# Whole rows by one indirect transfer, turned by sixteen VectorE transposes of 32 partitions

## The chip, the cores and the metric

The kernel runs on one core of one Trainium2 chip. The metric is device time in microseconds (us), the median of several runs. Engines are named as in the profile: PE is TensorE (its matmuls), PEld its weight loads, DVE is VectorE, ACT is ScalarE, POOL is GpSimd, SP is SyncE.

## The reference, cut to what matters

Three stages follow one another: a decaying linear attention, a dense feed-forward layer, and a layer of eight experts of which each token takes one. The change touches the third.

```python
x = attention(q, k, v, lam)                      # 1536 tokens x 512
h = x @ moe_w_in                                 # 512 -> 2048
x2 = np.maximum(0.01 * h, h) @ moe_w_out         # 2048 -> 512

logits = x2 @ w_gate + modality_bias[modality_id]
e_idx = np.argmax(logits, axis=1)                # one of 8 experts for each token
gate_w = softmax(logits)[np.arange(N), e_idx]
for e in range(8):
    mask = e_idx == e
    h = np.maximum(x2[mask] @ w1[e], 0.0)        # 512 -> 1024
    out[mask] = gate_w[mask, None] * (h @ w2[e]) # 1024 -> 512
```

Everything is 32-bit. Each large product is made of three matmuls, since every operand is split into a high part and the rest: `lo x hi`, `hi x lo` and `hi x hi`.

## The kernel before, in words

**Dense stage.** The 1536 tokens are three blocks of 512. For each block, 16 slices of 128 hidden features run through `layer1` and `layer2` on PE (12 matmuls of 128x512 each). Per slice, ACT makes the high parts of the weights (`split_in`, `split_out`) and of the activations (`hidden`), POOL the low parts of the weights, DVE the leaky ReLU and the low part of the activations (`leaky`). In the second half of the last block ACT and DVE also split the first expert's weights (`we_hi`, `we_lo`, L854 and L1219), one of 8 pieces per slice. The rows of x2 of a finished block are stored to DRAM, in `x2_d` (the profile calls it x_d); the router (`route`, `gates`, `slots`, `scatter_slots`) writes token numbers into `slots_d`, sorted by expert. `take` and `order` sort the experts.

**Expert stage.** It works on tiles of 128 tokens of one expert; here there are twelve, numbered 0 to 11, and three leftovers of at most 32 tokens of different experts, which are done together at the end (the mixed rows, names ending in `_m`). The first three tiles (`PRE`) belong to the first expert and take only tokens of the first two blocks; they are prepared while the dense stage ends. A tile t goes through this chain:

1. ACT's queue loads the token numbers (`load_rows`, L879), from tile 3 on.
2. POOL turns them into row addresses and issues the indirect transfer of the rows into `xg` (`gather`, `gather_early`).
3. DVE turns the rows so that features lie on the partitions, from `xg` into PSUM bank 6 (`turn_rows`, semaphore `s_et`).
4. ACT copies the high part out (`rows`, L800), DVE makes the low part (`rows_lo`, L1121).
5. PE multiplies: `up` twice (halves of 512 hidden features, 12 matmuls each), `turn_hidden` twice (L1493), `down` twice (12 matmuls each). ACT and DVE take the hidden features between them (`relu`, `hid`), DVE scales the result (`evacuate`) and POOL scatters it.

There is one `xg`, one bank for the turned rows, one `ids_n`. So tile t+1 can be gathered only after tile t is turned, and turned only after the low part of tile t is made. Each engine's order is written out by hand. On PE one body of the loop is `down(t, 0)`, `turn_hidden(t, 1)`, `up(t+1, 0)`, `down(t, 1)`, `turn_hidden(t+1, 0)`, `up(t+1, 1)`. On DVE it is `rows_lo(t+1)`, `hid(t, 1)`, `evacuate(t)`, `hid(t+1, 0)`, `turn_rows(t+2)`; in the body in which a new whole expert begins, sixteen halves of its weights' low parts are shared between DVE and POOL besides.

**Why the transpose is one instruction.** DVE's transpose turns blocks of 32x32 inside each group of 32 partitions. A full turn of 128 rows also has to bring rows of one partition group into another. The kernel before has the transfer do it: `x2_d` has four rows of 128 features for each token, one for each partition group, and the address of the row that partition p takes is four times the token number plus p // 32 (the constant `quarter`):

```python
pool.indirect_dma_start(out=xg[:, g * P:(g + 1) * P], ..., ap=ids_g[:, g:g + 1] ...)   # for g in 0..3
nc.vector.transpose(bank(T_PS).rearrange("p (c g j) -> p g c j", c=DC, g=QS),
                    xg[:].rearrange("p (g c i) -> p g c i", g=QS, c=DC))
```

For each g the 32 tokens of group g stand in all four partition groups, each time with another 128 of their features. That takes four indirect transfers of 128 pieces of 512 bytes, and four loads of token numbers.

Of the kernel before, what the change touches and what calls it, by code (L numbers as in the profile page):

```python
# [5 lines left out]
ALU = mybir.AluOpType  # L6
# [48 lines left out]
def fused_program(nc, attn_qk, attn_kv, lam, w_dense, modality, w_gate, mod_bias, w_exp, out):  # L55
# [6 lines left out]
    with ctx:  # L62
# [8 lines left out]
        x2_d = nc.dram_tensor("x2_d", [(TOK + 1) * QS, P], F32).ap()  # L71
        x2_rows = x2_d.rearrange("(t a) c -> t (a c)", a=QS)
# [103 lines left out]
        xg_m = place("xg_m", [P, MIX, P], F32)  # L176
# [15 lines left out]
        quarter = sb("quarter", [P, 1], F32)  # L192
# [29 lines left out]
        at_m = sb("at_m", [P, MIX], I32)  # L222
        at_m4 = sb("at_m4", [P, MIX], I32)
# [20 lines left out]
        at_pre = sb("at_pre", [P, PRE * QS], I32)  # L244
        at_pre4 = sb("at_pre4", [P, PRE * QS], I32)
        ids_n = sb("ids_n", [P, QS], I32)
        ids_g = sb("ids_g", [P, QS], I32)
# [4 lines left out]
        def bank(i):  # L252
            return psum[:, i, :]
# [143 lines left out]
        def _(sp):  # L397
# [84 lines left out]
            for t in range(BLOCKS):  # L482
# [3 lines left out]
                if t == BLOCKS - 1:  # L486
# [7 lines left out]
                    with nc.allow_non_contiguous_dma(reason="one id each"):  # L494
                        for a in range(QS):
                            sp.dma_start(at_pre[a * QR:(a + 1) * QR, :],
                                         slots_d[bass.ds(e_first * TOK, PRE * P), 0:1].rearrange("(g j) b -> j (g b)", j=QR)
                                         ).then_inc(s_idp, 16)
                sp.wait_ge(s_xr, DC * (t + 1))
                for a in range(QS):  # L500
                    sp.dma_start(x2_d[t * BLK * QS:(t + 1) * BLK * QS, :].rearrange("(b j a) n -> a j b n", a=QS, j=QR)[a],
                                 x2_r[a * QR:(a + 1) * QR].rearrange("p b c i -> p b (c i)")).then_inc(s_x2st, 16)
# [12 lines left out]
            for q in range(MIX):  # L515
                at = sp.value_load(m_tab[0:1, PLACES + q:PLACES + q + 1], min_val=0, max_val=SLOTS)
                sp.dma_start(ids_m[q * MR:(q + 1) * MR, :], slots_d[bass.ds(at, MR), :]).then_inc(s_mids, 16)
                with nc.allow_non_contiguous_dma(reason="one id each"):
# [23 lines left out]
        def _(pool):  # L542
# [14 lines left out]
            pool.dma_start(x2_rows[TOK:TOK + 1, :], zrow[:]).then_inc(s_out, 16)  # L557
# [56 lines left out]
            def gather_early(t):  # L614
                for g in range(QS):
                    pool.indirect_dma_start(out=xg[:, g * P:(g + 1) * P], out_offset=None, in_=x2_d[0:SURE * QS, :],
# [1075 lines left out]
```

## Time and profile before

| | |
|---|---|
| median of 3 runs | 521.85 us (521.41 to 525.5) |
| the profiled execution's own time | 522.88 us |
| its span in the trace | 521.0 us |
| PE busy | 484.8 us, 93% of the span |
| DVE busy | 202.9 us, 39% |
| ACT busy | 180.0 us, 35% |
| POOL busy | 247.8 us, 48% |
| mean granted TensorE clock | 0.982 of full speed |
| expert stage | from 329 us to the end |

The span runs from the first to the last instruction, and all times inside the program count from its start; the execution's own time holds 1.9 us more. A group in the profile is a line of the kernel with its engine and operation; where a row of the trace says `[x <-y]`, the engine sat idle for x us before it and y released it. The granted clock is 1.00 at 2.4 GHz and 0.50 at 1.2 GHz.

### The profile page before, as it was taken

What the parts mean: (1) busy time and instruction counts of PE and PEld (TensorE: products, weight loads), DVE (VectorE), ACT (ScalarE), POOL (GpSimd) and SP (SyncE); (2) the same over time, 40 slices, a digit from 0 to 9 for tenths busy, and PEclk for the clock granted to TensorE, in tenths of its full rate; (3) what the DMA queues carried; (4) which work ended last, traced back from release to release, by engine and by line L of the source; (5) the groups of instructions that cost most, each with busy time, mean ns of one, the idle gap of its engine ahead of it and who ended that gap; (6) DMA issues with size and microseconds to landing.
All of it is one profiled execution on the core that took longest, in us unless ns stands there. A gap on an engine that the chain in (4) does not pass through costs nothing.

```text
span 521.0 us, 8733 instructions
## 1 busy us (share of the span) xinstructions
PE 484.8 (93%) x2826; PEld 388.1 (74%) x2827; DVE 202.9 (39%) x434; ACT 180.0 (35%) x308; POOL 247.8 (48%) x265
## 2 busy tenths in 40 slices
PE   7899999999999999999999998879997988999991
PEld 6778888888778888877888886667775766888740
DVE  3533232333365422224632566466222372222210
ACT  0233334234354344445345555222221361222100
POOL 3874664554334556444446747361645175444300
PEclk9999999999999999999999999989998999999996
DMA  6954534321030620004700000400277728411100
GB/s 200 407 224 161 163 126 158 132 107 16 0 82 0 215 109 0 0 0 109 295 0 1 1 0 20 102 21 22 61 255 240 261 48 299 104 41 41 41 19 3
DMA packets 35433, 53.16 MB, mean 102 GB/s; under 512 B 15703, under 2 KB 23519, under 8 KB 35408
## 3 DMA queue, kind: packets, MB, share of 16 engines
q1 hardware_dynamic: 24576, 46.04, 26.7%
q0 software_dynamic: 3200, 6.77, 4.0%
q10 hardware_dynamic: 7632, 0.04, 0.8%
q8 instruction: 14, 0.23, 0.2%
q14 instruction: 11, 0.09, 0.1%
HBM read 46.41 MB, written 6.61 MB: 102 GB/s over the span
## 4 chain that ended last, share of the span: by engine, by line
PE 69%; DMA 7%; issue 7%; DVE 6%; ACT 4%; POOL 3%; ACTq 2%; POOLq 0%; SPq 0%; DVEq 0%
PE psum L1419 8%; PE psum L1427 7%; PE psum L1421 7%; PE psum L1420 7%; PE psum L1429 7%; PE psum L1428 7%; PE psum L1503 2%; PE psum L1382 2%; PE psum L1505 2%; PE psum L1504 2%; PE psum L1483 2%; PE psum L1377 2%; PE psum L1360 2%; PE psum L1485 2%; PE psum L1484 2%
## 5 line engine op out<-in xcount | busy, mean ns | idle before, releaser
L595 POOL TENSOR_TENSOR wi_lo<-wd_raw,wi_hi 128x512 fp32r<-128x512 f32 x48 | 62.1, 1294 | 138.2 <-ACT wi_hi L759 138.1
L1427 PE MATMUL psum<-act_lo,wo_hi 128*128 128x512 f32 x192 | 75.6, 394 | 2.4 <-DVE act_lo L1021 2.4
L1419 PE MATMUL psum<-xT,wi_lo 128*128 128x512 f32 x192 | 76.6, 399 | 0.0
L1421 PE MATMUL psum<-xT,wi_hi 128*128 128x512 f32 x192 | 74.9, 390 | 0.0
L1420 PE MATMUL psum<-xT,wi_hi 128*128 128x512 f32 x192 | 74.8, 390 | 0.0
L1429 PE MATMUL psum<-act_hi,wo_hi 128*128 128x512 f32 x192 | 74.8, 389 | 0.0
L1428 PE MATMUL psum<-act_hi,wo_lo 128*128 128x512 f32 x192 | 74.7, 389 | 0.0
L1018 DVE SCALAR_TENSOR_TENSOR act_f<-psum,act_f 128x512 f32<-128x512 f32 x48 | 33.1, 690 | 96.5 <-ACT act_f L777 96.0
L600 POOL TENSOR_TENSOR wo_lo<-wd_raw,wo_hi 128x512 fp32r<-128x512 f32 x48 | 61.9, 1289 | 1.0 <-ACT wo_hi L764 1.0
L777 ACT ACTIVATE act_f<-psum 128x512 f32<-128x512 f32 x48 | 28.7, 597 | 97.3 <-PE psum L1421 93.4
L696 POOL DMA_INDIRECT xg<-x_d,ids_g x40 | 41.0, 1025 | 18.4 <-issue 8.8
L1021 DVE TENSOR_TENSOR act_lo<-act_f,act_hi 128x512 fp32r<-128x512 f32 x48 | 35.5, 739 | 33.6 <-ACT act_hi L779 33.6
L1483 PE MATMUL psum<-we_hi,xe_lo 128*128 128x512 f32 x96 | 41.0, 427 | 6.1 <-DVE xe_lo L1121 4.2
L1427 PEld LDWEIGHTS psum<-act_lo,wo_hi 128*128 128x128 f32 x192 | 36.0, 188 | 12.6 <-issue 3.0
L779 ACT ACTIVATE act_hi<-act_f 128x512 fp32r<-128x512 f32 x48 | 30.4, 634 | 42.9 <-DVE act_f L1018 42.9
L1419 PEld LDWEIGHTS psum<-xT,wi_lo 128*128 128x128 f32 x192 | 36.0, 188 | 8.3
L1503 PE MATMUL psum<-we_hi,he_lo 128*128 128x512 f32 x96 | 38.8, 404 | 3.5 <-POOL we_lo L709 2.3
L1421 PEld LDWEIGHTS psum<-xT,wi_hi 128*128 128x128 f32 x192 | 36.0, 188 | 7.7
L1429 PEld LDWEIGHTS psum<-act_hi,wo_hi 128*128 128x128 f32 x192 | 36.0, 188 | 7.6
L1428 PEld LDWEIGHTS psum<-act_hi,wo_lo 128*128 128x128 f32 x192 | 36.1, 188 | 7.3
L1420 PEld LDWEIGHTS psum<-xT,wi_hi 128*128 128x128 f32 x192 | 36.1, 188 | 7.0
L1485 PE MATMUL psum<-we_hi,xe_hi 128*128 128x512 f32 x96 | 38.7, 403 | 0.0
(207 smaller groups left out, 742.4 us busy)
## 6 DMA issues: line engine op xcount, KB each, us to landing
we_raw<-w_exp SPq DMA_DIRECT2D x40, 512.0 KB, 5.2
wd_raw<-w_dense SPq DMA_DIRECT2D x16, 512.0 KB, 6.2
qk_in<-attn_qk SPq DMA_DIRECT2D x10, 512.0 KB, 3.4
kv_in<-attn_kv SPq DMA_DIRECT2D x10, 512.0 KB, 3.4
x_d<-x_r SPq DMA_DIRECT2D x12, 256.0 KB
qk_more<-attn_qk SPq DMA_DIRECT2D x2, 512.0 KB, 7.0
kv_more<-attn_kv SPq DMA_DIRECT2D x2, 512.0 KB, 7.8
ids_n<-slots_d ACTq DMA_DIRECT2D x44, 0.5 KB
```

The costliest lines, as they stand in the source:

```text
L595: nc.gpsimd.tensor_tensor(wi_lo[:, r, :], dense_raw(f, 0), wi_hi[:, r, :].bitcast(F32), ALU.subtract).then_inc(s_wil, 1)
L600: nc.gpsimd.tensor_tensor(wo_lo[:, r, :], dense_raw(f, 1), wo_hi[:, r, :].bitcast(F32), ALU.subtract).then_inc(s_wol, 1)
L696: pool.indirect_dma_start(out=xg[:, g * P:(g + 1) * P], out_offset=None, in_=x2_d, in_offset=bass.IndirectOffsetOnAxis(ap=ids_g[:, g:g + 1 ...
L1419: nc.tensor.matmul(h, w_lo, hi, start=(c == 0), stop=False)
L1420: nc.tensor.matmul(h, w_hi, lo, start=False, stop=False)
L1421: mm = nc.tensor.matmul(h, w_hi, hi, start=False, stop=(c == DC - 1))
L1427: nc.tensor.matmul(bank(ACC + c), hi, act_lo[:, r, :], start=first, stop=False)
L1428: nc.tensor.matmul(bank(ACC + c), lo, act_hi[:, r, :], start=False, stop=False)
L1429: return nc.tensor.matmul(bank(ACC + c), hi, act_hi[:, r, :], start=False, stop=last)
L1483: nc.tensor.matmul(bank(HID + half), xe_lo[:, c, :], w_hi, start=(c == 0), stop=False)
L1485: mm = nc.tensor.matmul(bank(HID + half), xe_hi[:, c, :], w_hi, start=False, stop=(c == DC - 1))
L1503: nc.tensor.matmul(bank(ACC), he_lo[:, f, :], we_hi[:, f, DM:], start=(f == 0), stop=False)
```

## The change

- `x2_d` has one row of 512 features for each token again. One indirect transfer of 128 pieces of 2 KB takes the place of four (also in `gather_early` and for the mixed rows), one load of token numbers takes the place of four, and a copy takes the place of the address arithmetic.
- `turn_rows` is sixteen transposes (`square`), each from one group of 32 partitions, g, to another, a. For the mixed rows it is twelve.
- The turn of tile 0 is moved into the last slices of the dense stage in two halves, `rows(0)` and `rows_lo(0)` before the last piece of the first expert's weights. Tile 1's turn is in two halves too, around `route` and `hid(0, 0)`.
- POOL issues the gather of tile 0 after the low parts that belong to slice 11; it stood ahead of the last low part of `wo` before.
- SP loads the weights of later experts once the gather of tile 3 is in; it no longer waits for token numbers too.

```diff
@@ SP
-                    with nc.allow_non_contiguous_dma(reason="one id each"):
-                        for a in range(QS):
-                            sp.dma_start(at_pre[a * QR:(a + 1) * QR, :], ...).then_inc(s_idp, 16)
...
-                    for a in range(QS):
-                        sp.dma_start(at_m[a * QR:(a + 1) * QR, q:q + 1], slots_d[bass.ds(at, MR), 0:1]).then_inc(s_mids, 16)
-
-            sp.wait_ge(s_gat, LOADS * (PRE + 1))
-            sp.wait_ge(s_ids, LOADS * (PRE + 1))
+            sp.wait_ge(s_gat, 16 * (PRE + 1))
@@ POOL
             def gather_early(t):
-                for g in range(QS):
-                    pool.indirect_dma_start(out=xg[:, g * P:(g + 1) * P], out_offset=None, in_=x2_d[0:SURE * QS, :], ...
+                pool.indirect_dma_start(out=xg[:], out_offset=None, in_=x2_d[0:SURE, :],
+                                        in_offset=bass.IndirectOffsetOnAxis(ap=ids_pre[:, t, 0:1].bitcast(U32), axis=0),
...
-            pool.wait_ge(s_x2st, LOADS * (BLOCKS - 1))
-            pool.wait_ge(s_chain, 8)
-            pool.wait_ge(s_idp, 16 + LOADS)
-            nc.gpsimd.tensor_scalar(at_pre4[:], at_pre[:], float(QS), quarter[:], ALU.mult, ALU.add).then_inc(s_chain, 1)
-            pool.wait_ge(s_chain, 9)
-            gather_early(0)
+            for i in range(FC1 - 6, FC1 - 2):
+                n = FC1 * (BLOCKS - 1) + i
+                split_in(n + 2, i + 2, i % 2)
+                split_out(n + 1, i + 1, 1 - i % 2)
+                if i == FC1 - 5:
+                    pool.wait_ge(s_x2st, LOADS * (BLOCKS - 1))
+                    pool.wait_ge(s_chain, 8)
+                    pool.wait_ge(s_idp, 16)
+                    gather_early(0)
             split_out(FC1 * BLOCKS - 1, FC1 - 1, 1)
...
             def gather(t):
-                nc.gpsimd.tensor_scalar(ids_g[:], ids_n[:], float(QS), quarter[:], ALU.mult, ALU.add).then_inc(s_idc, 1)
+                nc.gpsimd.tensor_copy(ids_g[:], ids_n[:]).then_inc(s_idc, 1)
...
-                for g in range(QS):
-                    pool.indirect_dma_start(out=xg[:, g * P:(g + 1) * P], out_offset=None, in_=x2_d, ...
+                pool.indirect_dma_start(out=xg[:], out_offset=None, in_=x2_d, ...
@@ ACT, last block, slices 8 to 15
                         hidden(n, i % 2)
+                        if i == FC1 - 1:
+                            rows(0)
                         ...
                         nc.scalar.activation(we_hi[:, f, :], we_raw[:, 0, f, :], ACT.Copy).then_inc(s_fh, 1)
-                    rows(0)
@@ DVE
-            def turn_rows(t):
-                dve.wait_ge(s_gat, LOADS * t + LOADS)
-                dve.sem_inc(s_pass, 1)
-                dve.wait_ge(s_exl, t)
-                nc.vector.transpose(bank(T_PS)..., xg[:]...).then_inc(s_et, 1)
+            def square(dst, src, a, g, count=QS):
+                return nc.vector.transpose(dst[a * QR:(a + 1) * QR].rearrange("p (c g j) -> p g c j", c=DC, g=count)[:, g],
+                                           src[g * QR:(g + 1) * QR].rearrange("p (a c i) -> p a c i", a=QS, c=DC)[:, a])
+
+            def turn_rows(t, part=range(QS)):
+                if 0 in part:
+                    dve.wait_ge(s_gat, 16 * t + 16)
+                    dve.sem_inc(s_pass, 1)
+                    dve.wait_ge(s_exl, t)
+                for g in part:
+                    for a in range(QS):
+                        ins = square(bank(T_PS), xg, a, g)
+                if QS - 1 in part:
+                    ins.then_inc(s_et, 1)
...
                     for i in range(FC2, FC1):
                         leaky(n0 + i, i % 2)
+                        if i == FC1 - 1:
+                            rows_lo(0)
                         dve.wait_ge(s_wol, n0 + i + 1)
                         dve.wait_ge(s_fh, i - FC2 + 1)
                         nc.vector.tensor_tensor(we_lo[:, i - FC2, :], we_raw[:, 0, i - FC2, :], ...).then_inc(s_first, 1)
-            turn_rows(0)
-            rows_lo(0)
+                        if i >= FC1 - 3 and i < FC1 - 1:
+                            turn_rows(0, range(2) if i == FC1 - 3 else range(2, QS))
             turn_x2(BLOCKS - 1)
             logit_parts(BLOCKS - 1)
-            turn_rows(1)
+            turn_rows(1, range(2))
             route(BLOCKS - 1)
             hid(0, 0)
+            turn_rows(1, range(2, QS))
             gates(BLOCKS - 1)
...
             hid(last, 1)
-            dve.wait_ge(s_mgat, 16 * MIX)
-            nc.vector.transpose(xT_m[:]..., xg_m[:]...).then_inc(s_mx, 1)
+            dve.wait_ge(s_mgat, 16)
+            for g in range(MIX):
+                for a in range(QS):
+                    ins = square(xT_m[:].rearrange("p c n -> p (c n)"), xg_m, a, g, MIX)
+            ins.then_inc(s_mx, 1)
```

In what follows, psum is the bank of PSUM that an instruction writes or reads, and a row without a count is one instruction. On DVE, at the end of the dense stage, from the leaky ReLU of slice 14 (act_f) on, the order before was:

```order
L1018 SCALAR_TENSOR_TENSOR act_f<-psum,act_f 128x512
L1021 TENSOR_TENSOR act_lo<-act_f,act_hi 128x512
L1219 TENSOR_TENSOR we_lo<-we_raw,we_hi 128x1024
L1018 SCALAR_TENSOR_TENSOR act_f<-psum,act_f 128x512
L1021 TENSOR_TENSOR act_lo<-act_f,act_hi 128x512
L1219 TENSOR_TENSOR we_lo<-we_raw,we_hi 128x1024
L1116 STREAM_TRANSPOSE psum<-xg 128x4x4x32
L1121 TENSOR_TENSOR xe_lo<-psum,xe_hi 128x512
L1096 STREAM_TRANSPOSE x_r<-psum 128x16x32 x4
```

Each slice there is act_f, act_lo and one piece of we_lo. After the change, from the squares ahead of the same slice 14 on:

```order
L1087 STREAM_TRANSPOSE psum<-xg 32x4x32 x8
L992 SCALAR_TENSOR_TENSOR act_f<-psum,act_f 128x512
L995 TENSOR_TENSOR act_lo<-act_f,act_hi 128x512
L1203 TENSOR_TENSOR we_lo<-we_raw,we_hi 128x1024
L1087 STREAM_TRANSPOSE psum<-xg 32x4x32 x8
L992 SCALAR_TENSOR_TENSOR act_f<-psum,act_f 128x512
L995 TENSOR_TENSOR act_lo<-act_f,act_hi 128x512
L1103 TENSOR_TENSOR xe_lo<-psum,xe_hi 128x512
L1203 TENSOR_TENSOR we_lo<-we_raw,we_hi 128x1024
L1070 STREAM_TRANSPOSE x_r<-psum 128x16x32 x4
```

Eight squares now stand ahead of the leaky ReLU of slice 14 and eight ahead of that of slice 15, and the low part of tile 0's rows ahead of the last piece of the first expert's weights. On DVE, at the end of a body of the expert loop without a new expert, the order before was:

```order
L1133 TENSOR_SCALAR y_sb<-psum,ids_s 128x512
L1126 ISA
L1127 TENSOR_TENSOR he_lo<-psum,he_hi 128x512
L1328 UNCONDITIONAL_BRANCH
L1113 ISA
L1116 STREAM_TRANSPOSE psum<-xg 128x4x4x32
```

And after the change:

```order
L1115 TENSOR_SCALAR y_sb<-psum,ids_s 128x512
L1108 ISA
L1109 TENSOR_TENSOR he_lo<-psum,he_hi 128x512
L1313 UNCONDITIONAL_BRANCH
L1092 ISA
L1087 STREAM_TRANSPOSE psum<-xg 32x4x32 x16
```

The place is the same and sixteen instructions stand where one stood. On POOL, around the end of the dense stage, before and then after:

```order
L674 TENSOR_SCALAR at_pre<-at_pre,quarter 128x12
L616 DMA xg<-x_d,at_pre 128x128 x4
L600 TENSOR_TENSOR wo_lo<-wd_raw,wo_hi 128x512
L616 DMA xg<-x_d,at_pre 128x128 x8
L606 DMA slots_d<-pairs,slot_i 12416x2 x4
```

```order
L580 TENSOR_TENSOR wi_lo<-wd_raw,wi_hi 128x512
L585 TENSOR_TENSOR wo_lo<-wd_raw,wo_hi 128x512
L600 DMA xg<-x_d,ids_pre 128x512
L580 TENSOR_TENSOR wi_lo<-wd_raw,wi_hi 128x512
L585 TENSOR_TENSOR wo_lo<-wd_raw,wo_hi 128x512
L580 TENSOR_TENSOR wi_lo<-wd_raw,wi_hi 128x512
L585 TENSOR_TENSOR wo_lo<-wd_raw,wo_hi 128x512 x2
L600 DMA xg<-x_d,ids_pre 128x512 x2
L591 DMA slots_d<-pairs,slot_i 12416x2 x4
```

The gather of tile 0 no longer stands between POOL and the last `wo_lo`, and those of tiles 1 and 2 are one transfer each.

## Rows read from the trace of the kernel before

**Rows 1.** Waits of PE from 320 us on: us in total, times, longest.

```profile
PE psum L1464 <- DVE seen_b L1067: 4.3, 1, 4.3
PE psum L1483 <- DVE xe_lo L1121: 4.2, 2, 3.5
PE psum L1503 <- POOL we_lo L709: 2.3, 1, 2.3
```

**Rows 2.** DVE groups, 280 us to the end: busy us, mean ns; idle before.

```profile
L1116 DVE STREAM_TRANSPOSE psum<-xg 128x512 f32<-128x512 f32 x13 | 9.4, 720 | 17.6 <-DMA xg<-x_d,ids_g 10.9 <-DMA xg<-x_d,at_pre 6.7
L1096 DVE STREAM_TRANSPOSE x_r<-psum 128x512 f32<-128x512 f32 x4 | 2.5, 682 | 0.0
```

**Rows 3.** DVE in order of time at the start: start us, us, instruction.

```profile
4.59 0.34 DVE L999 MEMSET quarter<- 32x1 f32 x4
4.98 0.06 DVE L1001 MEMSET e_down<- 128x1 f32 x1
4.99 0.06 DVE L1002 MEMSET e_slot<- 128x1 f32 x1
```

**Rows 4.** All engines in order of time, tile 3 from its turn to its first matmul.

```profile
369.85 0.73 DVE L1116 STREAM_TRANSPOSE psum<-xg 128x512 f32<-128x512 f32 x1 [3.13 <-DMA xg<-x_d,ids_g]
...
371.98 0.50 PE L1483 MATMUL psum<-we_hi,xe_lo 128*128 128x512 f32 x1 [0.70 <-DVE xe_lo L1121]
```

**Rows 5.** PE and DVE in order of time, an undisturbed body of the expert loop.

```profile
462.86 0.38 PE L1493 MATMUL psum<-ident,he 128*128 128x128 f32 x2
...
464.73 0.72 DVE L1116 STREAM_TRANSPOSE psum<-xg 128x512 f32<-128x512 f32 x1
...
474.70 0.60 PE L1493 MATMUL psum<-ident,he 128*128 128x128 f32 x4
```

**Rows 6.** PE in order of time: the loop's ends, and the first mixed matmuls.

```profile
377.56 0.38 PE L1493 MATMUL psum<-ident,he 128*128 128x128 f32 x2
...
486.55 0.38 PE L1493 MATMUL psum<-ident,he 128*128 128x128 f32 x2
...
494.73 0.42 PE L1619 MATMUL psum<-we_raw,xT_m 128*32 128x256 f32 x4
```

**Rows 7.** DVE and PE in order of time, end of the dense stage.

```profile
317.62 0.68 DVE L1018 SCALAR_TENSOR_TENSOR act_f<-psum,act_f 128x512 f32<-128x512 f32 x1
319.00 0.69 DVE L1021 TENSOR_TENSOR act_lo<-act_f,act_hi 128x512 fp32r<-128x512 f32 x1 [0.70 <-ACT act_hi L779]
320.54 1.23 DVE L1219 TENSOR_TENSOR we_lo<-we_raw,we_hi 128x1024 fp32r<-128x1024 f32 x1 [0.85 <-ACT we_hi L854]
...
325.95 0.47 PE L1427 MATMUL psum<-act_lo,wo_hi 128*128 128x512 f32 x1 [2.00 <-DVE act_lo L1021]
...
329.04 0.47 PE L1483 MATMUL psum<-we_hi,xe_lo 128*128 128x512 f32 x1
```

**Rows 8.** DVE in order of time, tables of the expert stage up to `hid(1, 0)`.

```profile
348.75 0.18 DVE L1238 TENSOR_TENSOR cnt_by<-at_rank,psum 1x64 f32<-1x64 f32 x1
...
353.71 0.67 DVE L1127 TENSOR_TENSOR he_lo<-psum,he_hi 128x512 fp32r<-128x512 f32 x1
```

**Rows 9.** Three stretches: length, busy us of PE, PEld, DVE, ACT, POOL; clock, DMA share, GB/s.

```profile
340.00:344.00 4.00, 2.34 (x15) 1.93 (x16) 3.65 (x17) 1.69 (x4) 2.77 (x3) 0.70 0.11 33
...
400.00:404.00 4.00, 3.00 (x7) 2.42 (x8) 1.38 (x2) 0.74 (x2) 2.94 (x3) 0.50 0.82 250
...
426.00:430.00 4.00, 2.59 (x11) 2.17 (x12) 1.42 (x2) 0.97 (x2) 3.98 (x5) 1.00 0.37 92
```

**Rows 10.** POOL and DVE in order of time, gather of tile 5 beside weight loads.

```profile
390.06 0.99 POOL L696 DMA_INDIRECT xg<-x_d,ids_g  x1 [0.89 <-POOL ids_g L690]
...
398.79 0.73 DVE L1116 STREAM_TRANSPOSE psum<-xg 128x512 f32<-128x512 f32 x1 [5.90 <-DMA xg<-x_d,ids_g]
```

**Rows 11.** DVE in order of time, the body in which a new expert begins.

```profile
413.92 0.69 DVE L1121 TENSOR_TENSOR xe_lo<-psum,xe_hi 128x512 fp32r<-128x512 f32 x1 [2.21 <-ACT xe_hi L800]
...
425.19 0.69 DVE L1109 TENSOR_TENSOR we_lo<-we_raw,we_hi 128x512 fp32r<-128x512 f32 x1 [0.35 <-issue]
```

More of the change, by code:

```diff
@@ L243, in fused_program @@
         ids_pre = sb("ids_pre", [P, PRE, 2], I32)
[L244 to L247, printed above, removed]
+        ids_n = sb("ids_n", [P, 2], I32)
+        ids_g = sb("ids_g", [P, 2], I32)
         ids_s = sb("ids_s", [P, 2], I32)
@@ L661, in _ @@
                 tail = t == BLOCKS - 1
-                for lo, hi in ((1, FC1 // 4), (FC1 // 4, FC1 // 2 - tail)):
+                for lo, hi in ((1, FC1 // 4), (FC1 // 4, FC1 // 2 - 3 * tail)):
                     with pool.Fori(lo, hi) as j:
@@ L694, in gather @@
                 pool.sem_inc(s_pass, 1)
-                for g in range(QS):
-                    pool.indirect_dma_start(out=xg[:, g * P:(g + 1) * P], out_offset=None, in_=x2_d,
-                                            in_offset=bass.IndirectOffsetOnAxis(ap=ids_g[:, g:g + 1].bitcast(U32), axis=0)
-                                            ).then_inc(s_gat, 16)
+                pool.indirect_dma_start(out=xg[:], out_offset=None, in_=x2_d,
+                                        in_offset=bass.IndirectOffsetOnAxis(ap=ids_g[:, 0:1].bitcast(U32), axis=0)
+                                        ).then_inc(s_gat, 16)
             def scatter(t):
@@ L717, in _ @@
             scatter_early(2)
-            pool.wait_ge(s_mids, (16 + LOADS) * MIX)
-            nc.gpsimd.tensor_scalar(at_m4[:], at_m[:], float(QS), quarter[:], ALU.mult, ALU.add).then_inc(s_chain, 1)
-            pool.wait_ge(s_chain, 10)
-            for q in range(MIX):
-                pool.indirect_dma_start(out=xg_m[:, q, :], out_offset=None, in_=x2_d,
-                                        in_offset=bass.IndirectOffsetOnAxis(ap=at_m4[:, q:q + 1].bitcast(U32), axis=0)
-                                        ).then_inc(s_mgat, 16)
+            pool.wait_ge(s_mids, 16 * MIX)
+            pool.indirect_dma_start(out=xg_m[0:MX, :], out_offset=None, in_=x2_d,
+                                    in_offset=bass.IndirectOffsetOnAxis(ap=ids_m[0:MX, 0:1].bitcast(U32), axis=0)
+                                    ).then_inc(s_mgat, 16)
             pool.wait_ge(s_tab, 1)
@@ L740, in _ @@
             pool.wait_ge(s_mout, 16)
-            pool.wait_ge(s_gat, LOADS * last + 2 * LOADS)
+            pool.wait_ge(s_gat, 16 * last + 32)
             pool.wait_ge(s_out, 16 * last + 32)
@@ L869, in _, with load_ids @@
             rows(1)
-            def load_ids(t):
+            def load_ids(dst, t, s):
                 slot = act.value_load(tab[0:1, bass.ds(SB_ + t, 1)], min_val=0, max_val=SLOTS - P)
-                act.dma_start(ids_s[:], slots_d[bass.ds(slot, P), :]).then_inc(s_ids2, 16)
-            def load_rows(t):
-                slot = act.value_load(tab[0:1, bass.ds(SB_ + t, 1)], min_val=0, max_val=SLOTS - P)
-                with nc.allow_non_contiguous_dma(reason="one id each"):
-                    for a in range(QS):
-                        act.dma_start(ids_n[a * QR:(a + 1) * QR, :],
-                                      slots_d[bass.ds(slot, P), 0:1].rearrange("(g j) b -> j (g b)", j=QR)).then_inc(s_ids, 16)
+                act.dma_start(dst[:], slots_d[bass.ds(slot, P), :]).then_inc(s, 16)
             hid(0, 1)
@@ L941, in _ @@
             act.sem_inc(s_pass, 1)
-            load_ids(last)
+            load_ids(ids_s, last, s_ids2)
             for q in range(MIX):
@@ L996, in finish @@
                                         ALU.subtract).then_inc(s_xl, 1)
-            for a in range(QS):
-                nc.vector.memset(quarter[a * QR:(a + 1) * QR, :], float(a))
             for e in range(E):
```

45 lines of the change are left out of this document (15 added, 30 removed).

## The prediction

> **What bounds the kernel now.** I read PE's waits first. PE is the engine with the most work, and from 320 us on it loses some 17 us in a few places: 4.3 us before the ranks, 4.2 us in two waits for the low part of a tile's rows, 2.3 us for a weight split on POOL [rows 1], and 2.0 us at the end of the dense stage [rows 7]. The two longest waits end with rows that arrive late: the gather of tile 5 takes from 390.06 to 398.79 us, 8.7 us, four transfers one behind another beside the weight loads [rows 10]. Each long wait also costs clock: in the stretch after either, the granted clock is 0.70 and 0.50 [rows 9], the lower of the two levels for part or all of it; PE was idle for 4.3 and 3.5 us ahead of them, while around the wait of 2.3 us, in the third stretch, it is 1.00. I put 1.2 us on the first fall and 2.4 us on the second: some six and twelve matmuls at 0.43 us each for 0.23.
>
> The rest of the expert stage is bound by PE. An undisturbed body takes 462.86 to 474.70, 11.84 us [rows 5]; DVE's transpose lies in the middle of it. So four transfers cost something in some bodies, and one transpose costs nothing in most. The change shortens the one and lengthens the other.
>
> **The square, which decides.** The transpose now takes 0.72 us for 512 elements of each partition [rows 2]. A square has 128. DVE's time grows by some 1.05 ns an element: 1.23 us for 1024 and 0.68 us for 512 [rows 7], so 384 fewer make 0.72 - 0.40 = 0.32 us. The question is what sixteen in a row take. Instructions that follow one another without a wait can overlap: four transposes in 2.5 us with 0.682 us for one start every (2.5 - 0.68) / 3 = 0.61 us [rows 2], so squares could start every 0.61 - 0.40 = 0.21 us, and a turn would be 15 x 0.21 + 0.32 = 3.4 us. Against that stand four memsets at the start, which write partitions 0 to 31, 32 to 63, 64 to 95 and 96 to 127 in turn. From 4.59 to 4.98 they and the step back take 0.39 us, 0.098 us each at 0.06 us of work, while the next two, which write from partition 0 on, start 0.01 us apart [rows 3]. So where the first partition of the output changes, an instruction waits for the one before to end, plus 0.04 us. In the squares the output's group changes each time. I take the held value, 0.32 + 0.04 = 0.36 us, and 15 x 0.356 + 0.32 = **5.7 us** for a turn, 2.8 us for a half; these rows are the nearest, though they write SBUF and not PSUM. The ends are 3.4 and 5.7 us.
>
> The Trainium skill ("VectorE: DVE Perf Modes", section "Two Vector instructions with no wait between them") says that an instruction is held until all earlier ones are done when the starting quadrant of its input or output differs from the last one in that memory. By that rule the turn is 5.7 us too; the memsets agree for the output side in SBUF, and no run here shows the input side.
>
> **Part 1, what becomes cheaper.** A gather is one instruction for four (1.0 us and 0.3 us between them, so 3.9 us off POOL), and three loads of token numbers of 0.4 us each leave ACT's queue. Both of PE's long waits go by this, and the 2.3 us too, for POOL comes to the weight split sooner. SP's small loads shrink and the weight loads start earlier; the last mixed weights have tens of us to spare. All this is inside the sums below, which take gathers as arrived unless said.
>
> **Part 2, end of the dense stage.** Before, DVE starts the leaky ReLU of slice 14 at 317.62 [rows 7]; act_lo follows 1.38 us later and takes 0.69. Now the first eight squares stand ahead: from 317.7 to 320.6. The leaky ReLU starts there, act_lo ends at 322.6, and PE, which wanted it at 321.1, waits 1.6 us. ACT splits after act_hi, so piece 6 of we_lo runs from 323.5 to 324.8, the second half of the squares to 327.6, act_lo of slice 15 to 329.7. PE starts the last `layer2` at 329.8 instead of 325.95 after 4.4 us of idling, and `up(0, 0)` 3.1 us later as before [rows 7]: **+3.8 us**. That POOL's gather is out of the way of `wo_lo` (the 2.0 us) doesn't help: the squares are late instead.
>
> **Part 3, tiles 0 to 2.** Let U be the start of `up(0, 0)`, 329.04 before. The gather of tile 1 is there in time now, so the first half of its turn runs from U + 3.4 to U + 6.2, `route` to U + 8.1, and the first `down` starts at U + 8.7 (U + 13.0 before). This is the large gain, 4.3 us, with the clock's 1.2. Then it is given back. The second half of the turn and `gates` stand ahead of `rows_lo(1)`: `up(1, 0)` at U + 13.6. The turn of tile 2 runs from U + 15.2 to U + 20.9, and the tables behind it; from the tables' start to `hid(1, 0)` are 4.96 us [rows 8] and 0.7 for itself, so `down(1, 0)` starts at U + 26.6, before U + 26.3, and PE idles 4.3 us. ACT's three loads fewer put `hid(1, 1)` back on time. The turn of tile 3 runs from U + 37.4 to U + 43.1. From the end of a turn to the first matmul are 370.58 to 371.98, 1.40 us [rows 4], so `up(3, 0)` starts at U + 44.5 against U + 42.9: **+1.6 us**.
>
> **Part 4, the loop.** Let P be the start of `turn_hidden(t+1, 0)`. DVE gets to the turn at P + 1.87 [rows 5] and ends it at P + 7.5; the next `up` starts at P + 8.9, and the next P is one `up` and one `down` later, 371.98 to 377.56, 5.58 us [rows 4, 6]: a body of **14.5 us** where PE's own work is 11.84. Eight bodies lie between 377.56 and 486.55, 109.0 us with their waits [rows 6]. Now they make 8 x 14.5 = 116.0. The body with a new expert is worse: DVE needs from 413.92 to 425.88, 12.0 us, from `rows_lo` to its last split [rows 11], and the turn stands behind that. By the same steps it and the next come to 32.8 us for 29.0. Together 119.8: **+10.8 us**.
>
> **Part 5, the end.** The turn after the last tile, which nothing needs, holds `hid(11, 1)` until P + 8.2, and twelve squares follow, 12 x 0.34 = 4.1 us, to P + 12.3. The mixed matmuls started at 494.73, P + 8.2 [rows 6]: **+4.1 us**.
>
> **Part 6, clock.** Idle stretches of 4.4 us (part 2), 4.3 us (part 3) and 4.1 us (the new expert) are as long as those behind which the clock fell. Three at the mean of 1.2 and 2.4 us: **+5.4 us**. The 2.65 us in each other body I leave at full clock, since 2.3 us did nothing.
>
> **Sum.** 3.8 + 1.6 + 10.8 + 4.1 + 5.4 = 25.7 us. On the profiled execution's 522.88 us this is 548.6, and on the median of the runs, 1.0 us lower, 547.6. I say **548 us**.
>
> **Rivals.** (a) *Squares overlap.* For it: transposes do overlap when all use the same partitions [rows 2], and the memsets have no input and don't write PSUM. At 3.4 us for a turn, the same steps give +1.7 at the dense end, -4.3 to tile 3, -7.1 in the loop (a body of 12.25 us, no waits for gathers), +0.5 at the end and +1.2 of clock: -8 us, **514 us**. The Trainium skill ("Vector Engine (DVE) Microarchitecture Reference", section 3.8) calls moves between quadrants free for up to 32 partitions; read as time, it is this case, and it would save 8 us. Chance 0.11.
> (b) *Only some are held*, those that also change the input's group, or the hold is shorter in PSUM. A turn of 4 to 4.9 us makes bodies of 12.8 to 13.7 us: 519 to 534 us. Chance 0.09; a third of it ends within 1%.
> (c) *The clock falls in the loop too*, because 2.65 us idle return every 14.5 us. Up to 2.4 us in each of eight bodies: 550 to 566 us. Chance 0.15. Against it, the wait of 2.3 us left the clock alone [rows 9].
> (d) *The change doesn't shorten the gathers*, since a transfer of 128 pieces of 2 KB moves the same bytes. It would matter little: a gather has from P + 7.5 to the next P + 1.9, which is 8.9 us, about the 8.7 us of tile 5 [rows 10]. So it adds 0 to 3 us inside the forecast.
>
> **How the numbers follow.** The forecast with the clock as in part 6 has 0.65, at 536 to 556: the low end has a turn of 5.1 us (no 0.04 us between squares, 0.55 us off eleven turns) and two falls of the clock fewer, the high end four falls more of 1.8 us. With (c) this is 0.80. The range of 8 in 10 reaches into (b) and most of (c): 528 to 560. The chances: a run of this kernel can be told from no change from about 1% on, 5 us. Faster is (a) with a bit of (b), 0.12; within 1% 0.05; slower 0.83. The point from which the change loses is a turn of about 3.9 us, 0.24 us for a square.
>
> **What would show it.** DVE's transposes with 32 partitions take about 0.32 us each and start 0.36 us apart, a turn 5.7 us; some 220 of them add about 60 us of DVE time, 203 to 260 us and more. Bodies of PE are 14.5 us, each with a wait of some 2.6 us for xe_lo. PE waits 4 us for act_lo before the last `layer2`, and 4 us for he_lo before `down(1, 0)`. No gather is waited for on DVE. The wait for seen_b is gone. The prediction is wrong if squares start 0.21 us apart, or if the clock goes to its lower level in the loop.

## The result and the profile after

The changed kernel takes **550.17 us** (median of 4 runs, 549.39 to 550.83) against 522.07 us for the kernel before in the same session: 1.052 times as long, 95% interval 1.048 to 1.057. The forecast was 548 us. The profiled execution took 549.39 us, its span is 547.7 us and its mean granted clock 0.969.

First the squares. Two groups of DVE over the whole span, each with its total busy time and the mean ns of one:

```profile
L1087 DVE STREAM_TRANSPOSE psum<-xg 32x128 f32<-32x128 f32 x208 | 67.1, 323 | 4.2 <-DMA xg<-x_d,ids_pre 1.2
L1087 DVE STREAM_TRANSPOSE xT_m<-xg_m 32x128 f32<-32x128 f32 x12 | 3.6, 301 | 0.1
```

Then DVE in order of time in a plain body of the loop, the place of [rows 5]:

```profile
400.86 0.75 DVE L1115 TENSOR_SCALAR y_sb<-psum,ids_s 128x512 f32<-128x512 f32 x1 [4.78 <-PE psum L1492]
401.82 0.69 DVE L1109 TENSOR_TENSOR he_lo<-psum,he_hi 128x512 fp32r<-128x512 f32 x1 [0.21 <-ACT he_hi L790]
402.54 5.37 DVE L1087 STREAM_TRANSPOSE psum<-xg 32x128 f32<-32x128 f32 x16
408.57 0.69 DVE L1103 TENSOR_TENSOR xe_lo<-psum,xe_hi 128x512 fp32r<-128x512 f32 x1 [0.66 <-ACT xe_hi L782]
```

Sixteen squares of 0.323 us fill 5.37 us and the last takes 0.33 us, so one starts every (5.37 - 0.33) / 15 = 0.336 us. They stand end to end with 0.01 us between them, where the single transpose of [rows 2] took 0.72 us. The last row starts 6.0 us after the squares' start, and PE waits for it. The waits of PE from 315 us on, in the place of [rows 1]:

```profile
PE psum L1470 <- DVE xe_lo L1103: 22.6, 9, 5.6
PE psum L1414 <- DVE act_lo L995: 5.0, 2, 4.1
PE psum L1490 <- DVE y_sb L1115: 4.7, 1, 4.7
PE psum L1470 <- DVE we_lo L1078: 3.4, 1, 3.4
PE psum L1606 <- DVE xT_m L1087: 2.0, 1, 2.0
PE psum L1490 <- DVE he_lo L1109: 1.9, 2, 1.4
```

All of them end with DVE. Those for `seen_b` and for the split on POOL are gone, and so is DVE's wait for gathers, but for 1.2 us early on. The sum is 39.6 us where the kernel before idled some 17 us. In the rows that follow, a P is the start of `turn_hidden` for the first half of a tile, as in the prediction. PE in order of time at its key places, those of [rows 6] and [rows 7]: the last `layer2`, `up(3, 0)`, the P of the loop's first body and of its last, and one wait in the loop:

```profile
329.27 0.77 PE L1414 MATMUL psum<-act_lo,wo_hi 128*128 128x512 f32 x1 [4.07 <-DVE act_lo L995]
...
378.94 0.50 PE L1470 MATMUL psum<-we_hi,xe_lo 128*128 128x512 f32 x1 [2.23 <-DVE xe_lo L1103]
...
386.14 0.60 PE L1480 MATMUL psum<-ident,he 128*128 128x128 f32 x4
...
409.40 0.49 PE L1470 MATMUL psum<-we_hi,xe_lo 128*128 128x512 f32 x1 [2.31 <-DVE xe_lo L1103]
...
512.96 0.49 PE L1480 MATMUL psum<-ident,he 128*128 128x128 f32 x3
```

The eight bodies take 512.96 - 386.14 = 126.8 us where they took 109.0 [rows 6]. And the clock, in four stretches around or behind a wait of 2.2 to 2.3 us each (length, busy us of PE; granted clock, DMA share, GB/s):

```profile
378.00:382.00 4.00, 3.06 (x10) 0.78 0.82 259
394.00:398.00 4.00, 3.02 (x13) 1.00 0.72 259
462.00:466.00 4.00, 4.00 (x12) 0.57 0.21 60
476.00:480.00 4.00, 3.05 (x13) 1.00 0.25 66
```

The waits are alike, yet two stretches stay at the upper level (2.4 GHz), and two go to the lower one (1.2 GHz) for part of the time.

### The profile page after: what moved, and what is told of

It is laid out like the page before. It is cut to its first block, busy times and chain, and to the rows that moved or that the text cites. A ratio compares the mean times of both kernels' runs of the same rounds, so it can differ in the third digit from the quotient of the medians.

```text
span 547.7 us, 8758 instructions
## 1 busy us (share of the span) xinstructions
PE 493.5 (90%) x2826; PEld 393.6 (72%) x2827; DVE 265.4 (48%) x636; ACT 180.8 (33%) x308; POOL 205.0 (37%) x222
## 4 chain that ended last, share of the span: by engine, by line
PE 68%; DVE 19%; ACT 5%; issue 4%; DMA 2%; DVEq 0%; SPq 0%; ACTq 0%; POOL 0%; POOLq 0%
DVE psum L1087 12%; PE psum L1406 7%; PE psum L1414 7%; PE psum L1416 7%; PE psum L1415 7%; PE psum L1408 7%; PE psum L1407 7%; PE psum L1470 3%; PE psum L1347 2%; PE psum L1369 2%; PE psum L1472 2%; PE psum L1471 2%; PE psum L1490 2%; PE psum L1364 2%; PE psum L1492 2%
## 5 line engine op out<-in xcount | busy, mean ns | idle before, releaser
L992 DVE SCALAR_TENSOR_TENSOR act_f<-psum,act_f 128x512 f32<-128x512 f32 x48 | 33.1, 690 | 96.4 <-ACT act_f L759 96.0
L1087 DVE STREAM_TRANSPOSE psum<-xg 32x128 f32<-32x128 f32 x208 | 67.1, 323 | 4.2 <-DMA xg<-x_d,ids_pre 1.2
L1470 PE MATMUL psum<-we_hi,xe_lo 128*128 128x512 f32 x96 | 43.2, 450 | 26.1 <-DVE xe_lo L1103 22.6
L995 DVE TENSOR_TENSOR act_lo<-act_f,act_hi 128x512 fp32r<-128x512 f32 x48 | 33.7, 702 | 33.6 <-ACT act_hi L761 33.6
L1470 PEld LDWEIGHTS psum<-we_hi,xe_lo 128*128 128x128 f32 x96 | 19.7, 205 | 32.7 <-issue 21.9
```

The lines of the kernel that those rows point to most:

```text
L995: nc.vector.tensor_tensor(act_lo[:, r, :], act_f[:, r, :], act_hi[:, r, :].bitcast(F32), ALU.subtract).then_inc(s_gl, 1)
L1087: return nc.vector.transpose(dst[a * QR:(a + 1) * QR].rearrange("p (c g j) -> p g c j", c=DC, g=count)[:, g], src[g * QR:(g + 1) * QR].rea ...
L1470: nc.tensor.matmul(bank(HID + half), xe_lo[:, c, :], w_hi, start=(c == 0), stop=False)
```

## The experiments

In each session the kernel before ran beside them: 519.2 us with the first four, 519.5 us with the next four, 520.6 and 517.7 us with the last two pairs. A time without an interval is of one run; the runs of the kernel before in the first session lay between 516.2 and 521.0 us, so a few us between such times say nothing. Kernels 2, 3 and 7 leave out the move of rows between groups, in all or some turns; their transfers, tiles and matmuls are the same.

**1. The input's group changes each time.** The loops over the squares change places.

```
-                for g in part:
-                    for a in range(QS):
+                for a in part:
+                    for g in range(QS):
```

> The same sixteen squares in another order, so that the output's group of partitions changes only with every fourth square and the input's with each. If an instruction is held where either of the two changes, squares still start 0.336 us apart, a turn stays at 5.4 us and the time at about 550 us. If the output's group alone decides (all that the memsets of the kernel before could show), three of four squares start about 0.21 us apart, a turn takes 3.9 us and the time is about 520 us.

Measured 551.36 us. DVE in order of time, the same turn as above:

```profile
404.21 5.37 DVE L1087 STREAM_TRANSPOSE psum<-xg 32x128 f32<-32x128 f32 x16
```

Nothing has changed. Here the output stays in its group in three of four steps, and the squares are still end to end. In the changed kernel it is the input that stays. So a change on either side alone takes the overlap away, with the output in PSUM and the input in SBUF.

**2. Squares that stay in their group.** The rows are left in the group of partitions that they are in.

```
-                        ins = square(bank(T_PS), xg, a, g)
+                        ins = nc.vector.transpose(bank(T_PS)[g * QR:(g + 1) * QR, a * P:(a + 1) * P],
+                                                  xg[g * QR:(g + 1) * QR, a * P:(a + 1) * P])
```

> Sixteen squares of the same size, but each read and written in one and the same group of partitions, which changes with every fourth; the rows are not moved across groups. If the change of group is what holds a square, twelve of sixteen starts are about 0.21 us apart and four 0.336, a turn takes 3.9 us and the time is about 520 us. If squares of 32 partitions never overlap, a turn stays at 5.4 us and the time at 550 us.

Measured 529.8 us. The turn of tile 4 on DVE, and a later first matmul of a body on PE:

```profile
382.38 3.66 DVE L1097 STREAM_TRANSPOSE psum<-xg 32x128 f32<-32x128 f32 x16
...
449.68 0.49 PE L1471 MATMUL psum<-we_hi,xe_lo 128*128 128x512 f32 x1 [0.61 <-DVE xe_lo L1104]
```

Sixteen squares in 3.66 us, one every 0.22 us on the mean: they do overlap when the group stays. In the trace the starts in this turn are 0.24, 0.19 and 0.19 us apart inside the first group and 0.29 us at the change to the next, where the square ahead took 0.27: only the three squares that change the group start as the one before ends. Nor is it the move of rows across groups that holds a square: here nothing moves across, and in the changed kernel the squares that stay in their group start 0.33 to 0.34 us after the one before, like the rest. The hold by a change of group from one square to the next is therefore the cause of the 5.4 us, not the small size or the 32 partitions. But the time is 10 us above what I expected of such a turn; the section on the prediction says why.

**3. One transpose in place of sixteen squares.**

```
-                for g in part:
-                    for a in range(QS):
-                        ins = square(bank(T_PS), xg, a, g)
+                if QS - 1 in part:
+                    ins = nc.vector.transpose(bank(T_PS).rearrange("p (c g j) -> p g c j", c=DC, g=QS),
+                                              xg[:].rearrange("p (g c i) -> p g c i", g=QS, c=DC))
```

> The cheaper gather alone: one transfer of whole rows and one transpose over 128 partitions for a tile; the move across groups is left out. If the squares are the whole loss, the time is below the kernel before by what the three other transfers cost: bodies of 11.84 us, no wait for a gather, no fall of the clock in the loop, about 508 us. If the single gather brings nothing, 520 us.

Measured 500.32 us, 19 us below the kernel before, and 50 us below the changed kernel. PE's waits from 310 us on, all of them:

```profile
PE psum L1606 <- DVE xT_m L1087: 1.7, 1, 1.7
PE psum L1490 <- DVE he_lo L1109: 0.9, 2, 0.5
PE psum L1470 <- DVE xe_lo L1103: 0.8, 1, 0.8
PE psum L1414 <- DVE act_lo L995: 0.4, 1, 0.4
```

The single gather is worth more than I gave it: 3.8 us of waits are left of some 17, and the clock doesn't fall before the end. The squares on DVE eat this and 31 us more.

**4. The turn elsewhere in the body.** In a plain body it goes ahead of the wait for the tile's sum, and the mixed squares ahead of the last low part. In the body with a new expert it stays last.

```
                     split2(k1, 7, raw_of(k1))
+                    turn_rows(t + 2)
                 with dve.Else():
                     hid(t, 1)
+                    turn_rows(t + 2)
                     evacuate_late(t)
                     hid(t + 1, 0)
-                turn_rows(t + 2)
-            hid(last, 1)
             dve.wait_ge(s_mgat, 16)
...
             ins.then_inc(s_mx, 1)
+            hid(last, 1)
```

> The same squares, but in the loop the turn of the tile after next stands behind the first thing of the body and ahead of the wait for the tile's sum, where DVE waits some 4 us in the trace, and the mixed rows are turned ahead of the last low part. If a turn costs PE only by where it stands, plain bodies fall from 14.4 to 11.9 us with no wait for xe_lo and the clock stays up in them: about 536 us, since the dense end, tiles 0 to 2 and the new expert's body keep their loss. If DVE's 5.4 us more of work are too much for a body anyway, bodies stay above 13 us and the time above 545 us.

Measured 538.29 us, 1.038 times the kernel before (1.033 to 1.044). The expected time is nearly met, the expected reason isn't. DVE in order of time, the longest wait and one of a plain body, and POOL ahead of each:

```profile
396.93 0.18 POOL L676 COPY ids_g<-ids_n 128x2 int32<-128x2 int32 x1 [6.65 <-DMA ids_n<-slots_d]
...
403.17 5.37 DVE L1087 STREAM_TRANSPOSE psum<-xg 32x128 f32<-32x128 f32 x16 [7.03 <-DMA xg<-x_d,ids_g]
...
469.32 1.01 POOL L688 DMA_INDIRECT out<-y_sb,ids_s  x1 [9.54 <-DVE y_sb L1115]
...
474.91 5.37 DVE L1087 STREAM_TRANSPOSE psum<-xg 32x128 f32<-32x128 f32 x16 [0.94 <-DMA xg<-x_d,ids_g]
```

Now the turn is early enough for PE, but the gather isn't there. DVE waits 14.4 us for gathers in all, in six places, of three kinds. Four waits in plain bodies, of 0.9 to 1.4 us and 4.2 us together, are for a gather that is issued behind the scatter of the tile before, which waits for the `y_sb` that the turn holds up. The wait of 7.0 us is not of that kind: POOL had waited 6.65 us for the load of the token numbers. And that of 3.2 us, at 449.6 us, is for a gather that had to wait until the turn before it, in the new expert's body, was through with `xg`.

**5. The gather ahead of the scatter.** As 4; in plain bodies ACT loads the next token numbers first, and POOL gathers before it scatters.

```
-                gather(t + 2)
...
-                scatter(t)
+                    scatter(t)
+                    gather(t + 3)
+                with pool.Else():
+                    gather(t + 3)
+                    scatter(t)
```

> The kernel with the moved turn, in which DVE then waited up to 7 us for a gather; here the loads of the token numbers and the gather of the tile after next come ahead of the scatter, so that a gather has a whole body. If the late gather is what kept the moved turn at 538 us, the waits for gathers go from 14 us to under 3, plain bodies come to 11.9 us and the time to about 530 us; the dense end, tiles 0 to 2 and the new expert keep their loss, so it stays slower than before. If it stays at 538 us, DVE's added work is the limit itself.

Measured 533.47 us (ratio 1.025, 1.018 to 1.032). PE in order of time, three turns of the hidden rows, two for each body:

```profile
481.33 0.60 PE L1485 MATMUL psum<-ident,he 128*128 128x128 f32 x4
487.26 0.60 PE L1485 MATMUL psum<-ident,he 128*128 128x128 f32 x4
493.18 0.60 PE L1485 MATMUL psum<-ident,he 128*128 128x128 f32 x4
```

493.18 - 481.33 = 11.85 us: a plain body is as short as before, with all sixteen squares in it. The four short waits of kernel 4 are gone. DVE still waited 8.9 us for gathers, in the two places that have another cause: 5.6 us up to the turn at 401.5 us and 3.3 us up to that at 447.9. So the expected 530 us were missed by 3. What is left of the loss lies ahead of the loop and in the new expert's body, which this edit doesn't touch.

**6. PE turns the rows.** Four transposes on PE for each tile replace the squares; the first weights are laid out to match on the way in. The mixed rows keep their twelve squares on DVE, ahead of the last low part as in 4.

```
+            def turn_rows(t):
+                pe.wait_ge(s_gat, 16 * t + 16)
+                pe.sem_inc(s_pass, 1)
+                pe.wait_ge(s_exl, t)
+                for a in range(QS):
+                    mm = nc.tensor.transpose(bank(T_PS)[:, a * P:(a + 1) * P], xg[:, a * P:(a + 1) * P], ident[:])
+                mm.then_inc(s_et, 1)
...
                 turn_hidden(t + 1, 0)
+                turn_rows(t + 2)
...
-        "w_exp": np.concatenate([moe2_w1.reshape(E, DC, P, 2, HF).transpose(0, 3, 1, 2, 4).reshape(E * FC2, P, HF),
+        "w_exp": np.concatenate([moe2_w1.reshape(E, DC, QS, QR, 2, HF).transpose(0, 4, 2, 1, 3, 5).reshape(E * FC2, P, HF),
```

> Rows come whole by one transfer, as in the changed kernel, but PE turns them: four transposes of 128 partitions and 128 columns for each tile, as it turns the hidden rows, with the experts' first weights laid out to match on the way in. PE gets some 0.36 us more for each of eleven tiles, 4 us in all, and DVE loses its turns. If the squares on DVE are the whole loss of the changed kernel, this lands near the kernel with one DVE transpose for a tile (500.3 us) plus 4 us: about 504 us, faster than both kernels. If PE has to wait for the gather instead, because it reaches the turn earlier than DVE did, 510 to 520 us.

Measured **509.26 us**, 0.979 of the kernel before (0.972 to 0.985): faster than both. PE's waits for gathers from 300 us on, and the longest of them:

```profile
PE psum L1463 <- DMA xg<-x_d,ids_g: 4.9, 3, 4.0
...
388.11 1.04 PE L1463 MATMUL psum<-ident,xg 128*128 128x128 f32 x4 [4.04 <-DMA xg<-x_d,ids_g]
```

The expected 504 us were missed by these waits. A body takes 12.29 us, so a turn costs PE 12.29 - 11.84 [rows 5] = 0.45 us and not 0.36.

**7. Squares ahead of the loop only.** In the loop `turn_rows(t + 2, whole=True)` does one transpose, as in 3.

> Squares for tiles 0 to 4 and the mixed rows, one transpose over 128 partitions for each tile turned in the loop (their rows stay in their groups). From 550 us down to 500 us there are 50 us for twelve turns that are 4.65 us longer. If the loop has lost what the traces show (bodies 17.8 us, the end 3.6 us, and the 8 us of gathers that one transfer would have saved there), this comes to about 522 us. If what the early turns lose is only pushed on, more than 530 us.

Measured 522.18 us, as expected. Of the 50 us between 3 and the changed kernel some 28 belong to the turns in the loop and 22 to the five ahead of it. (The mixed rows are squares in both.)

**8. The kernel before with four transposes for one.** Each has 128 partitions and 128 elements.

```
-                nc.vector.transpose(bank(T_PS).rearrange("p (c g j) -> p g c j", c=DC, g=QS),
-                                    xg[:].rearrange("p (g c i) -> p g c i", g=QS, c=DC)).then_inc(s_et, 1)
+                for g in range(QS):
+                    ins = nc.vector.transpose(bank(T_PS).rearrange("p (c g j) -> p g c j", c=DC, g=QS)[:, g],
+                                              xg[:].rearrange("p (g c i) -> p g c i", g=QS, c=DC)[:, g])
+                ins.then_inc(s_et, 1)
```

> The kernel before, with each tile's transpose cut in four of 128 partitions and 128 elements each, which all start at partition 0. If only a change of partition group holds an instruction, they start about 0.21 us apart and a turn takes 0.95 us for 0.72: the time stays within 1% of the kernel before. If short transposes are slow to start whatever the group, they start 0.33 us apart, a turn takes 1.3 us and the time is still within 1 to 2%.

Measured 520.01 us. One turn of the loop:

```profile
473.50 0.89 DVE L1117 STREAM_TRANSPOSE psum<-xg 128x128 f32<-128x128 f32 x4
```

At 0.29 us for one, a start every (0.89 - 0.29) / 3 = 0.20 us. Cutting the transpose up cost next to nothing here, where all the pieces start at the same partition. Each piece writes PSUM in the same four runs of 32 as a square of the changed kernel does, so that pattern doesn't hold an instruction either.

**9 and 10. Earlier gathers for kernel 6.** As in 5, in all bodies: ACT loads the next numbers first, and POOL has `gather(t + 3)` ahead of `scatter(t)`; kernel 6 runs once more beside it.

> The kernel in which PE turns the rows, with the token numbers of a tile loaded and its rows gathered ahead of the scatter before it, as in the run with the moved gather. In the trace without this, PE waits 4.0 us at 388.1 us for the gather of tile 5 and 0.7 us at 428.0, and the long wait costs clock (some 1.4 us). If those waits are the gather's place in the queues, they go and the time is 5 to 6 us lower, about 504 us. If the load of the numbers lands late whatever its place (6 us beside the weight loads), nothing changes: 509 us.

> The kernel in which PE turns the rows, once more, on the same chip as the one with earlier gathers, so that the two can be compared: 509 us, and waits of PE for a gather of some 5 us again.

Measured 513.3 us for the earlier gathers (0.986, 0.982 to 0.990) and 509.55 us for kernel 6 (0.977, 0.972 to 0.981). The guess was wrong. Two of POOL's waits in the first:

```profile
POOL ids_g L676 <- DMA ids_n<-slots_d: 46.3, 8, 8.6
POOL xg L681 <- DVE y_sb L1105: 17.7, 5, 4.1
```

POOL now sits up to 8.6 us at the copy of the token numbers, with the scatter queued behind it. PE still waits 2.5 us for one gather, and 3.1 us for `he` from ACT. In kernel 6 POOL's waits for the token numbers sum to 14.7 us. But the two profiled executions took 510.69 and 510.81 us, as good as the same, so these waits don't explain the 3.7 us between the medians; their cause stays open.

**11 and 12. The waits filled.** In the changed kernel ten matmuls that nobody reads stand ahead of each `up(t + 1, k_next, 0)` of the loop; the changed kernel runs once more beside it.

```
+                for _ in range(10):
+                    nc.tensor.matmul(bank(MISC)[:, 0:P], ident[:], ident[:], start=True, stop=True)
                 up(t + 1, k_next, 0)
```

> The changed kernel, with ten matmuls of 128 columns that nobody reads put in front of each first expert layer in the loop, in the place where PE otherwise idles 2.3 us for the low part of the rows. If PE's idle stretches are what lets the clock fall in three of seven plain bodies, PE idles well under 1 us there, the clock stays at its upper level in them, and the time falls by the three times 1.6 us that the falls cost: about 545 us for 550. If the ten take longer than the wait, bodies grow and it is slower than 550 us; if the clock falls for another reason, 550 us with the same falls.

> The changed kernel once more, on the same chip as the one with the filled waits: 550 us, waits of 2.3 us in seven plain bodies, with the clock falling behind some of them. If the falls are a matter of chance, they come in other bodies than in the first trace.

Measured 545.99 us with the waits filled and 551.9 us without (ratios to the kernel before 1.052, 1.047 to 1.057, and 1.064, 1.059 to 1.069). PE in order of time, and three stretches of the filled kernel behind them:

```profile
393.07 0.60 PE L1480 MATMUL psum<-ident,he 128*128 128x128 f32 x4
393.50 2.40 PE L1591 MATMUL psum<-ident 128*128 128x128 f32 x20
395.98 0.49 PE L1470 MATMUL psum<-we_hi,xe_lo 128*128 128x512 f32 x1
```

```profile
394.00:398.00 4.00, 3.92 (x27) 1.00 0.99 333
462.00:466.00 4.00, 3.92 (x23) 1.00 0.25 66
476.00:480.00 4.00, 3.92 (x25) 1.00 0.26 66
```

The ten take just the time of the wait (the timeline lists them as 20 pieces), `up` starts when its rows are there, and all six plain bodies of the loop take 14.4 us. In the kernel beside it three of six take 16.0. That is 4.8 us of clock; the medians are 5.9 us apart. These falls come behind PE's idling and go with it. Which of the equal waits brings one is another matter: in the first trace of the changed kernel it was those ending at 378.94, 460.93 and 505.77 us, in the second those at 395.95, 478.42 and 508.85, and in kernel 1 those at 395.02, 462.87 and 507.71.

## Why the prediction was right, and where it was not

It held by its main step, the held squares, and by errors that cancelled: the clock cost 5.4 us more than predicted, the shorter squares and steps took 1.1 us off, and 3.3 us went at the end of the span, where no term stood. That 548 us came so near to 550.17 is to that extent luck. Its own steps, in us of the profiled executions:

| Term | predicted | measured |
|---|---|---|
| a turn | 5.7 | 5.37 |
| part 2, to `up(0, 0)` | +3.8 | +4.6, of it 1.2 clock |
| part 3, U to the first P of the loop | +1.6 | +4.0, of it 3.2 clock |
| part 4, eight bodies | +10.8 | +17.8, of it 6.4 clock |
| part 5, end | +4.1 | +3.6 |
| part 6, clock | +5.4 | inside the rows above, 10.8 |
| behind the mixed matmuls | 0 | -3.3 |
| sum | 25.7 | 26.7 |

**The square.** 0.32 us was right (0.323). The choice of the held value was right, and kernels 1, 2 and 8 show the hold directly. The gap of 0.04 us, from the memsets of [rows 3], was too large: it is 0.01. The Trainium skill ("VectorE: DVE Perf Modes", section "Two Vector instructions with no wait between them") names the starting quadrant of input or output as what holds an instruction; kernel 1 agrees for the input alone and the changed kernel for the output alone, at 0.336 us a start against the 0.22 us of kernel 2.

**Parts 2 and 3.** The last `layer2` starts at 329.27, predicted 329.8. From U = 333.60 the first `down` starts at U + 8.3 (predicted 8.7), `up(1, 0)` at U + 12.7 (13.6), `down(1, 0)` at U + 26.3 (26.6) and `up(3, 0)` at U + 45.3 (44.5). PE idled 4.7 us ahead of `down(1, 0)`, where I had 4.3, and the 1.6 us of clock that this wait costs are part of the last number: without them it is U + 43.7.

**Part 4.** A plain body takes 14.4 us, predicted 14.5: the waits are 2.3 us, not 2.65. Without its clock the loop takes 120.4 us, predicted 119.8. The pair of bodies around the new expert was 33.9 us without clock, for 32.8 predicted.

**Part 6 was the mis-sized term.** "The 2.65 us in each other body I leave at full clock, since 2.3 us did nothing": one row of the kernel before, where the clock stayed up, was taken as a rule. Three of seven waits of 2.3 us brought a fall of 1.6 us, and so did the waits of 4.7, 3.4 and 5.6 us; the fall behind that of 4.1 us cost 1.2 us. Seven falls and 10.8 us, not three and 5.4: rival (c) came true in part, and so did the prediction's own sign of being wrong, a clock that goes to its lower level in the loop. Squares 0.3 us shorter for each turn and the next term made up for it.

**The term that I didn't have.** From the first mixed matmul to the end of the span the changed kernel takes 22.9 us, and the kernel before 26.3. The last scatter is issued alike; what follows is shorter. The last scatter of kernel 8, whose span is 518.0 us:

```profile
508.17 0.95 POOL L737 DMA_INDIRECT out<-y_m,ids_m  x1 [5.84 <-DVE y_m L1344]
```

That leaves 9.8 us behind its issue, as in the kernel before (9.75 us). In the changed kernel (541.27 to 547.7) and all its variants it is 6.4 to 6.5 us. The timeline ends there, but the trace holds one more long instruction of POOL: once the scatter has landed, 2.7 us after its issue, a DRAIN fills the rest of the span. It takes 6.695 us in the kernel before and in kernel 8, 3.339 us in the changed kernel. Its length goes with the number of indirect transfers that POOL has issued in the whole program. There are 80 in those two kernels and 39 in the changed one and most variants; kernels 5 and 9 issue 40, and theirs takes 3.421 us. That is 0.082 us for each transfer in all fourteen traces, and 41 transfers fewer give the 3.36 us. What the engine does in that time isn't shown.

**The rivals.** (a) and (b) fell with kernels 1 and 2, and (a) also had the wrong price. At 3.4 us for a turn it gave 514 us, and kernel 2, at 3.66 us, took 529.8. Its plain bodies are 12.7 us, near the 12.5 that my steps give. But the turn of tile 5 still waited 2.1 us for its gather, so that body took 16.3 us with its fall of the clock. The new expert's pair took 33.1 us where the rival's sum leaves 109.0 - 7.1 - 6 x 12.25 = 28.4. And up to the loop it lost 2.8 us where the steps gave a gain of 2.6. So the break-even was off too. I put it at a turn of 3.9 us; a straight line between kernels 3 (0.72 us, 500.3 us) and 2 crosses the 519.2 us of the kernel before at 2.6 us. The low end of the range was added up wrong besides: eleven turns 0.55 us shorter and two falls of 1.8 us fewer make some 538 us, not 536. (d) didn't come up: no gather was waited for in the loop of the changed kernel, since its bodies are so long. Kernels 4 to 6, with shorter bodies, did wait for gathers, up to 7 us.

**Part 1 was too small.** I listed what the single gather takes away and then took it as inside the other sums. Kernel 3 puts it at 19 us by the runs, together with the new order of work at the end of the dense stage, which no run takes apart from it. Against the profiled execution of the kernel before, the path to the loop's first P is 9.1 us shorter, the eight bodies 11.6 us, and what follows them 1.7 us, although the DRAIN alone is 3.4 us shorter; PE now waits 1.7 us for the twelve mixed squares.

## What to carry to other kernels

Ask of an engine's row of small instructions not only what one takes but whether the next may start inside it: a few neighbouring rows of the same trace that differ in the partition they start at showed the answer here before the change was made. A cheaper transfer that is paid for on another engine should be placed with it: the same squares cost 28 us in the loop at one place, and 17 of the whole went when they and the gather stood elsewhere, and the engine with the better-suited operation (PE, 0.45 us for a turn) made a gain of 2% out of a loss of 5%. And price the idle time of PE with its clock, for one wait that left the clock up says little about the next seven.

## What the runs showed that I had not expected

- Equal waits of PE, 2.3 us behind equal work, brought a fall of the clock three times of seven in each of three traces, in different bodies. Each costs 1.6 us. Matmuls that nobody reads, put into the waits, removed all of them and were worth about 5 us.
- Squares over 32 partitions start 0.22 us apart on the mean where the group changes with every fourth (0.19 to 0.24 us inside a group), and 0.336 us where it changes each time, on either side alone.
- POOL waited up to 8.6 us for the load of 128 token numbers, 1 KB, in kernel 9. Issuing the loads and gathers earlier made that kernel slower, by 3.7 us in the medians.
- The DRAIN of POOL that ends the program is 0.082 us longer for each indirect transfer that it has issued: 3.4 us between four gathers a tile and one.
